# q and k of the last four attention tiles turned during the first batch, kept in device memory and loaded back

## What is computed

```python
for c in range(nc):                                   # attention, chunk = 32
    k_full = np.concatenate([mem_k, k_ctx], axis=2)   # 8 memory rows and the window
    v_full = np.concatenate([mem_v, v_ctx], axis=2)
    scores = scale * np.matmul(q_c, k_full.transpose(0, 1, 3, 2))
    a = softmax(scores)
    out[:, :, c_start:c_end] = np.matmul(a, v_full)
x = out as (3072, 512)
h = x @ w_in                                          # 512 -> 1024
solu = h * softmax(h)
ln = (solu - mean) / sqrt(var + 1e-6) * g_ln
x2 = ln @ w_out                                       # 1024 -> 512
h = x2 @ moe2_w_in                                    # 512 -> 2048
out = (h * clip(h + 3, 0, 6) / 6) @ moe2_w_out
```

## Time and profile before

| | us |
|---|---|
| median of 3 runs (908.24 to 909.01) | 908.4 |
| the profiled execution: its own time | 907.72 |
| the profiled execution: its span | 905.6 |
| first batch, to the first `project` | 0 to 73.7 |
| attention and first layer, with what overlaps them | 73.7 to about 410 |
| second layer | to the end |

### The profile page before, as it was taken

How to read it: one execution, slowest core, us unless ns; L and a number is a source line. 1 busy time by engine, 2 the same in 40 slices (tenths; PEclk the granted TensorE clock), 3 DMA queues, 4 the chain that set the end, 5 groups by cost and what they waited for, 6 DMA issues and landing times.

```text
span 905.6 us, 16510 instructions
## 1 busy us (share of the span) xinstructions
PE 887.2 (98%) x6144; PEld 794.8 (88%) x6144; DVE 676.9 (75%) x1100; ACT 470.7 (52%) x1092; POOL 265.9 (29%) x327
## 2 busy tenths in 40 slices
PE   7899999999999999999999999999999999999998
PEld 6778888888888888899888888888799999999998
DVE  5998878888777878757685555555898987979784
ACT  6666565656565565627574555455654333333321
POOL 4392554563431453450112233223510000000000
PEclk9999999999999999999999999999999999999999
DMA  9744266656554574558633323333997435354341
GB/s 206 167 96 107 57 187 177 187 155 184 148 153 119 149 214 123 190 205 314 253 126 140 128 104 139 134 142 117 337 351 268 145 95 162 95 162 140 117 140 47
DMA packets 147196, 146.70 MB, mean 162 GB/s; under 512 B 96952, under 2 KB 107704, under 8 KB 146104
## 3 DMA queue, kind: packets, MB, share of 16 engines
q1 hardware_dynamic: 133539, 100.29, 38.3%
q0 software_dynamic: 7920, 38.94, 11.9%
q10 hardware_dynamic: 5669, 6.56, 2.1%
HBM read 90.05 MB, written 55.71 MB: 161 GB/s over the span
## 4 chain that ended last, share of the span: by engine, by line
PE 85%; DVE 8%; DMA 3%; ACT 1%; issue 1%; SPq 0%; ACTq 0%; POOL 0%; DVEq 0%; POOLq 0%
PE banks L981 26%; PE banks L1270 23%; PE banks L1029 23%; PE banks L926 3%; PE banks L955 2%; PE banks L934 2%; PE banks L896 2%; PE banks L972 2%; PE banks L996 2%; DMA gs_raw<-g_scratch 2%; DVE prob L1640 1%; DVE gs L1601 1%; DVE small L1618 1%; DVE score L1610 1%; DVE gs_raw L1954 1%
## 5 line engine op out<-in xcount | busy, mean ns | idle before, releaser
L1270 PE MATMUL banks<-vs,gs 128*128 128x256 f32 x2016 | 242.9, 283 | 1.1 <-DVE o_stage L1998 0.7
L1270 PEld LDWEIGHTS banks<-vs,gs 128*128 128x128 f32 x2016 | 242.2, 192 | 1.8 <-DVE o_stage L1998 0.9
L1029 PE MATMUL banks<-xs,ws 128*128 128x512 f32 x1008 | 231.2, 390 | 0.6 <-DVE part L1729 0.3
L1029 PEld LDWEIGHTS banks<-xs,ws 128*128 128x128 f32 x1008 | 188.0, 188 | 42.5 <-issue 2.0
L1558 ACT CAST gs<-gs_raw 128x1792 fp32r<-128x1792 f32 x48 | 81.4, 1697 | 125.7 <-DVE gs_raw L1954 125.7
L981 PE MATMUL banks<-y_t,w_out 128*128 128x384 f32 x768 | 140.9, 338 | 0.0
L981 PEld LDWEIGHTS banks<-y_t,w_out 128*128 128x128 f32 x768 | 132.2, 188 | 0.7
L981 PE MATMUL banks<-w_in,x_t 128*128 128x512 f32 x480 | 114.5, 394 | 0.0
L1337 ACT ACTIVATE prob<-score,small 96x128 f32<-96x128 f32 x256 | 99.3, 392 | 16.6 <-DVE small L1618 16.1
L1954 DVE TENSOR_TENSOR gs_raw<-gs_raw 128x256 f32<-128x256 f32 x192 | 82.2, 429 | 31.6 <-DMA gs_raw<-g_scratch 26.8
L981 PEld LDWEIGHTS banks<-w_in,x_t 128*128 128x128 f32 x480 | 88.6, 188 | 18.7
(11 more groups left out here) (94 smaller groups left out, 1071.1 us busy)
## 6 DMA issues: line engine op xcount, KB each, us to landing
g_scratch<-part SPq DMA_DIRECT2D x96, 256.0 KB, 2.0
gs_raw<-g_scratch SPq DMA_DIRECT2D x45, 512.0 KB, 3.8
q_in<-in_q_dram SPq DMA_DIRECT2D x32, 192.0 KB, 4.4
x_scratch<-x_out ACTq DMA_DIRECT2D x32, 192.0 KB, 2.7
k_in<-in_k_dram SPq DMA_DIRECT2D x24, 240.0 KB
v_in<-in_v_dram SPq DMA_DIRECT2D x24, 240.0 KB
out_dram<-o_stage SPq DMA_DIRECT2D x11, 512.0 KB, 5.4
v_split_scratch<-v_split POOLq DMA_DIRECT2D x3, 1792.0 KB, 8.0
```

The lines of the kernel that those rows point to most:

```text
L1029: mm = pe.matmul(ps, ws[:, W_OF[i], a, kc, :], xs[g][X_OF[i]][:, m, kc, :], start=(fresh and x == 0), stop=(x == len(passes) - 1), skip_gr ...
L1270: mm = pe.matmul(m_ps[i][:, s, :], gs[x][:, a, G_OF[i], s * P:(s + 1) * P], vs[p][:, m, V_OF[i], :], start=(p == 0 and s == 0 and y == 0), ...
```

## The change

Tiles 28 to 31, the last four of the last batch, are called ahead (`is_ahead`, AHEAD = 4, e = 0 to 3). During the first batch SP loads their q and k into two slots of new buffers `q_raw` and `k_raw`, PE transposes them into bank 7 (`turn_ahead_q`, `turn_ahead_k`), ACT copies them out (`copy_ahead_q`, `copy_ahead_k`), and SP stores the turned tiles in device memory (`keep_ahead`). In the last batch SP loads the turned tiles into `q_back` and `k_back`, which lie where `q_in` and `k_in` lie, `scores` reads them from there, and `turn_qk` and `copy_qk` of these four tiles are gone. The first batch's orders are written anew on all five engines, and `keep_busy` has 23 matmuls there where it had 24. Five semaphores of fixed values become one (`fixed_ready`).

```diff
             def load_q(b, t):
                 n = TILES * b + t
-                if type(n) is not int or n >= 2:
+                if n >= 2 and is_ahead(n - 2):
+                    sp.wait_ge(scores_done, 2 * n - 2)
+                elif n >= 2:
                     sp.wait_ge(qk_turned, 2 * n - 3)
+                if is_ahead(n):
+                    sp.dma_start(q_back[t % 2][:, :, :], q_dram[n - NA + AHEAD]).then_inc(q_in_here[t % 2], 16)
+                    return
...
+            def load_ahead_q(e):
+                t = ahead_tile(e)
+                if e >= 2:
+                    sp.wait_ge(ahead_turned, 2 * e - 3)
+                sp.dma_start(q_raw[:, e % 2], q[B - 1, :, TQ * t:TQ * (t + 1), :].rearrange("h s d -> s h d")
+                             ).then_inc(raw_here[e % 2], 16)
+
+            def load_ahead_k(e):
+                if e >= 2:
+                    sp.wait_ge(ahead_turned, 2 * e - 2)
+                load_window(sp, k_raw, k, mem_k, raw_here, B - 1, ahead_tile(e))
+
+            def keep_ahead(e):
+                sp.wait_ge(ahead_copied, 2 * e + 2)
+                sp.dma_start(q_dram[e], q_ahead[:, e % 2]).then_inc(ahead_kept[e % 2], 16)
+                sp.dma_start(k_dram[e], k_ahead[e % 2][:, :, :]).then_inc(ahead_kept[e % 2], 16)
...
+                load_ahead_q(3)
+                keep_ahead(1)
+                keep_ahead(2)
+                load_ahead_k(3)
+                keep_ahead(3)
...
+            def turn_ahead_q(e):
+                pe.wait_ge(raw_here[e % 2], raw_count(e))
+                turn(ahead_ps, q_raw[:, e % 2], TQ, ahead_turned)
+
+            def turn_ahead_k(e):
+                turn(ahead_ps, k_raw[:, e % 2], NK, ahead_turned)
...
                 pe.wait_ge(y_lo_done, 2 * (turned_tile(i, 0) + [0, 1, 1, 2][u]))
+                if is_ahead(n):
+                    return
...
                 attend(0, 6, False)
+                pe.wait_ge(ahead_copied, 7)
+                turn_ahead_k(3)
                 pe.wait_ge(y_lo_done, 5)
                 pe.wait_ge(y_lo_done, 6)
+                pe.wait_ge(ahead_copied, 8)
...
-                    if not last:
+                    if not last and not is_ahead(n + 1):
                         copy_qk(n + 1)
```

More of the change, by code:

```diff
@@ L344, in work, with is_ahead, ahead_tile, raw_count @@
             }
+        IDENT_READY, THREE_READY, MASK_READY = 2, 3, 5
+        def is_ahead(n):
+            return n >= NA - AHEAD
+        def ahead_tile(e):
+            return TILES - AHEAD + e
+        def raw_count(e):
+            return 16 * sum(1 + LOADS[ahead_tile(x)] for x in range(e % 2, e + 1, 2))
+        def k_in_count(n):
+            b, t = n // TILES, n % TILES
+            return kv_here(b, t) - (16 * sum(LOADS[x] - 1 for x in range(TILES - AHEAD, t + 1) if x % 2 == t % 2) if is_ahead(n) else 0)
         def first_cols(m):
@@ L455, in _ @@
             for b in range(1, B):
+                if b == B - 1:
+                    for s in range(2):
+                        sp.wait_ge(ahead_kept[s], 16 * AHEAD)
                 batch(b)
@@ L835, in _ @@
             first_batch()
+            for s in range(2):
+                pool.wait_ge(ahead_kept[s], 16 * AHEAD)
             batch(1, steps=0, start=1)
@@ L892, in _, with turn @@
         def _(pe):
-            def turn(ps, src, width):
+            def turn(ps, src, width, turned=qk_turned):
                 for c in range(KD):
@@ L898, in turn @@
                                         ident[0:width, 0:width])
-                last.then_inc(qk_turned, 1)
+                last.then_inc(turned, 1)
             def turn_q(t, ps):
@@ L939, in turn_probs @@
                 for half in range(2):
-                    if behind_qk:
+                    if behind_qk and not is_ahead(n + 1):
                         pe.wait_ge(qk_copied, 2 * n + 3 + half)
-                    elif half == 0:
+                    elif not behind_qk and half == 0:
                         pe.wait_ge(y_lo_done, 2 * MPG * (NG - 1))
@@ L1113, in first_batch @@
                 turn_q(5, turn_ps[0])
+                turn_ahead_q(0)
                 hidden_part(1, 0)
                 hidden_part(1, 1)
-                hidden_part(1, 2)
                 pe.wait_ge(prob_copied, 8)
                 turn_k(5, turn_ps[1])
+                hidden_part(1, 2)
                 hidden_part(1, 3)
                 attend(0, 3, False)
-                scores(5, False)
                 pe.wait_ge(qk_copied, 11)
                 turn_half(4, 0)
+                scores(5, False)
+                pe.wait_ge(ahead_copied, 1)
+                turn_ahead_k(0)
                 pe.wait_ge(qk_copied, 12)
@@ L1133, in first_batch @@
                 hidden_part(2, 2)
-                hidden_part(2, 3)
                 pe.wait_ge(y_lo_done, 1)
                 turn_q(6, turn_ps[0])
+                hidden_part(2, 3)
                 pe.wait_ge(y_lo_done, 2)
                 turn_k(6, turn_ps[1])
+                pe.wait_ge(ahead_copied, 2)
+                turn_ahead_q(1)
+                attend(0, 4, False)
                 pe.wait_ge(qk_copied, 13)
@@ L1156, in first_batch @@
                 hidden_part(3, 3)
-                scores(7, False)
                 pe.wait_ge(qk_copied, 15)
@@ L1161, in first_batch @@
                 turn_half(6, 1)
+                scores(7, False)
                 pe.wait_ge(prob_copied, 13)
```

301 lines of the change are left out of this document (178 added, 123 removed).

## The result

| kernel | median | lowest to highest | runs |
|---|---|---|---|
| before | 908.7 us | 907.27 to 912.25 | 6 |
| changed | 916.61 us | 915.73 to 919.59 | 6 |

The ratio is 1.009, with a 95% interval of 1.0074 to 1.0105. The change makes the kernel 7.9 us slower; 5.0 were forecast. Direction and range held, and the size was 3 us low.

The account below looks back on a forecast made before the run. PE was taken as the bound, busy 98% of the span, with the first batch more DVE's. -3.1 + 1.0 + 0.4 + 1.6 + 5.1 = +5.0 us on 907.7 gave 912.7, as median 913.4 us; range 909 to 918.

Parts of the forecast that it names:

- taken out: Last batch, tiles 28 to 31: PE time without the q and k transposes falls by 3.1 us, bounds 2.2 to 3.3.
- ahead transposes, exposed: First batch: 1.0 us of six transpose groups exposed on PE, plus 0.4 for q of ahead tile 3.
- first wait: Before q of ahead tile 3: PE waits 1.6 us for k of ahead tile 3 to land, between 0 and 3.
- second wait: First batch's end: tile 8's loads, issued behind the ahead stores, make PE's k 5.1 us late, between 4.5 and 7.
- new order: First batch: rewritten engine orders and four more loads in full DMA queues, costed at 0, between -2 and +2 us.
- clock: Behind the second wait: PE's granted clock stays as it is, costing 0; this forecast got chance 0.52.
- rival 1: PE's clock falls behind the second wait, slowing `project`: +2.2 us, 915.6 us, up to 918; chance 0.22.
- Rival 2: First batch: the new order takes out 4 us of DVE's waiting, giving 906.8 us; chance 0.14.
- Rival 3: Last batch: the gain is lost, for example to late loads or DVE, giving 916.5 us; chance 0.06.
- Near 80: Sign at the first batch's end: the first `project` begins near 80 us instead of 73.7.

Follow-up runs that it names:

- f3: Kernel before, no ahead work put in, last batch as in the changed kernel but loading back stored zeros: 906.43 us, ratio 0.9974.
- e2: Changed kernel, loads of tile 8's q and k ahead of ahead tiles 2 and 3's stores, ahead tile 3's k ahead of all stores: 907.57 us, ratio 0.9992.
- e4: Changed kernel's new order on all engines, with all ahead work taken out and the last batch as before: 910.83 us, ratio 1.0024.
- e5: Changed kernel with the load of k of ahead tile 3 issued ahead of the stores of ahead tiles 1 and 2: 915.20 us, ratio 1.0071.
- e3_fill_wait: Changed kernel with 16 idle matmuls on PE behind the last ahead copy, before q of tile 8: 917.17 us, ratio 1.0091.
- e1_tile8_first: Changed kernel with loads of q and k of tile 8 issued ahead of the stores of ahead tiles 2 and 3: 911.69 us, ratio 1.0039.
- f4_wait_moved: f1_old_order_ahead with PE's wait for the last ahead copy moved from before q of tile 8 to before `project`: 907.92 us, ratio 0.9991.
- f1_old_order_ahead: Kernel before, its old order kept, with the ahead work put in and the last batch as changed: 907.79 us, ratio 0.9984.

## Why the prediction was right, and 3 us low

Term by term, each measured in single profiles, as a difference of two kernels that differ in little but that term:

| term | forecast | measured | from |
|---|---|---|---|
| taken out | -3.1 | -3.2 | attention stretch, f3 and e2 against before |
| ahead transposes, exposed | 1.0 + 0.4 | 1.7 | stretch, e2 - e4 |
| first wait | 1.6 | 1.6 | stretch, changed - e5 |
| second wait | 5.1 | 5.5 (0.4 of it the clock's) | stretch, e5 - e2 |
| new order | 0 | 1.6 | stretch, e4 - before |
| clock | 0 (rival 1: 2.2) | 1.0, and the 0.4 above | `project`, 5.43 - 4.43 |
| sum | 5.0 | 8.2 | 7.9 in whole runs |

The whole runs by themselves give: order 2.2, the work put in and taken out -2.9 (e2 against e4; the terms give 1.7 - 3.2 = -1.5), first wait 1.7, second wait with clock 7.2, together 8.2 us. Either sum closes by construction, since each kernel is subtracted from the next on the way from before to changed; only the single terms can be compared, and in whole runs each is uncertain by about 1.5 us or more.

**Taken out: right.** The step of tile 31 is 1.02 us shorter; 0.92 were forecast. With the slow `project` taken off, the changed kernel's attention stretch is 294.9 us, as in f3 and e2. What came back later can't be seen: f3 is 2.4 us faster in whole runs, with 3.2 within its interval.

**The first wait: right in its mechanism, its size in part by luck.** The chain that the prediction laid from the end of `turn_ahead_k(2)` to the landing was 5.1 us. In the trace that transpose ends about 68.5 and q is turned at 73.66: 5.1 us. PE had 3.4 us to do in it and waited 1.76. But e3_fill_wait, with the same list, took 5.9 us and waited 2.54, and in e1_tile8_first the wait is 3.19, each with the clock down behind it; taking the first wait away was worth 1.7 us of whole runs beside the second wait (changed against e5) and 4.1 without it (e1 against e2).

**The second wait: right in its mechanism and, in part by luck, in its size.** ACT and SP in the changed kernel, against the earlier trace rows:

```profile
79.75 1.07 ACT L1442 CAST y_t<-banks 128x512 fp32r<-128x512 f32 x2 [0.72 <-PE banks L1050]
80.71 1.13 ACT L1468 ACTIVATE h_exp<-banks,small 128x1024 f32<-128x1024 f32 x1
...
81.81 0.60 ACT L1424 COPY k_ahead<-banks 128x512 f32<-128x512 f32 x1
```

```profile
82.44 0.34 SPq L474 DMA_DIRECT2D q_ahead_scratch<-q_ahead  x1
82.82 0.43 SPq L475 DMA_DIRECT2D k_ahead_scratch<-k_ahead  x1
83.30 0.45 SPq L446 DMA_DIRECT2D q_in<-in_q_dram  x1
...
84.73 0.50 SPq L408 DMA_DIRECT2D k_in<-in_k_dram  x1
```

The chain from the casts is the one forecast: `exp_hidden(3)` 1.13 us, the copy 0.60, two stores 0.86, then the loads. The last piece of k went out 1.43 us behind q (1.18 forecast) and landed some 3.3 us later (2.8 forecast): 0.8 us more than the working had. As a difference of two kernels the wait comes to 5.5 us. It is not more, because e2_both_first, from which it is counted, turns k of tile 8 itself 0.7 us later behind ACT's casts than before did (2.15 us against 1.46), waiting for the last ahead copy. And 0.4 of the 5.5 are the clock's: from k of tile 8 to `project` are 0.77 us (88.09 to 88.86) where they are 0.36 in e2_both_first.

**The clock: the step that failed.** The forecast took the clock as it is at 0.52 and rival 1 at 0.22. Rival 1 holds: at 1.00 before the wait, 0.50 behind it, in the changed kernel and in e5_k3_first; with the wait filled, 1.00. The argument against it, that the trace of before shows no fall, was worth little, since PE is never idle there for more than 1.54 us behind its start, as the prediction itself says, and so it was no test of a wait of 5. With the 0.4 us on k of tile 8 the fall cost 1.4 us in the changed kernel's profile and 2.3 in e5_k3_first's (`project` 6.34 us), against the 2.2 of rival 1; in the changed kernel the clock comes back within `project`. No whole run shows this cost by itself, since e3_fill_wait came out no faster.

**The new order: the term that was mis-sized.** It was costed at 0, between -2 and +2, and it costs 1.6 us in the stretch and 2.2 in whole runs (0.7 to 3.7 by the interval). The 0 was the middle between two guesses, less waiting of DVE and later loads; what decides, where in its list PE meets DVE, was in neither. e4_order_only shows these meetings at 41.09, 50.35 and 64.18. Which engine's list makes them late is not shown: POOL's order and one transpose of PE were tried alone and changed nothing. Rival 2, that the new order pays, falls with it.

**The ahead transposes: nearly right.** 1.7 us for 1.4; in the old order 2.3, of which 0.5 is the wait for the last copy (f4_wait_moved against f1_old_order_ahead).

**The rest.** Rival 3 is refuted by the attention stretch; that its 916.5 us is nearly the measured time is luck, and so is rival 1's 915.6 in part, as it has no cost of the order. The first `project` begins at 88.86 us. "Near 80" was a slip of the prediction's: its own terms put 8.1 us ahead of it, which gives 81.8. Of the 7.0 us between, 2.3 are the terms that were too small and 4.8 the late start of this one profile, most of it the scaling of 3.83 us on DVE. No experiment ties it to the change, as the eight other profiles with the new order start at 36.34 to 38.75. What part of the start is the change's own is not settled; profiles of one execution each can't tell it.

Put together: of 8 us lost, 6.5 are one line too late in SP's list, with what the clock adds to it, 1.6 are another line there, and the rest of the change is about level: the order and the work put in cost 3.2 us and the work taken out gives 3.2 back.

## What to carry to other kernels

A queue that issues DMAs in order makes every load behind a waiting store as late as the store; a load with a deadline belongs ahead of it, and for a step that is moved the whole list of the issuing engine has to be read, not only that of the engine that computes. Work that is moved out of a full stretch into a less busy one gains its length and costs what the holes there don't hold, here 3.2 us against 1.7 for the work and 1.6 for the order written to make room for it. An idle time longer than any in the profile at hand should be priced with a fall of the clock behind it; here that was 1.4 and 2.3 us in two profiles.

## What the runs showed of the hardware that I had not expected

The clock also falls behind shorter idle times, in the first 38 us, where the DMA queues are full. In the changed kernel PE is idle for 2.56 us before 22.50 and for 3.34 us before 31.58:

```profile
22.50 0.87 PE L969 MATMUL banks<-ident,k_in 128*128 128x128 f32 x4 [2.56 <-DMA k_in<-in_k_dram]
...
31.58 0.52 PE L1022 MATMUL banks<-ident,prob 96*128 96x96 f32 x4 [3.34 <-DVE prob L1765]
```

```profile
8.00:38.00 30.00, 21.76 (x188) 18.78 (x189) 26.34 (x43) 17.55 (x71) 14.32 (x18) 0.89 1.11 236
20.00:24.00 4.00, 1.50 (x9) 1.53 (x10) 3.93 (x8) 1.84 (x9) 1.56 (x2) 0.84 1.13 270
```

Here no single idle time has to be that long. In f3_take_out_only, which has the old order, PE is idle for 1.42 us before 22.11 and for 1.49 before 26.12, the longest between 8 and 38 us, and no longer than the 1.54 us of before, behind which the clock stayed at 1.00. Yet it falls (time line of PE, then a window):

```profile
26.12 0.52 PE L1025 MATMUL banks<-ident,prob 96*128 96x96 f32 x4 [1.49 <-DVE prob L1743]
...
28.34 2.02 PE L1017 MATMUL banks<-k_t,q_t 64*96 64x128 f32 x16
```

```profile
28.00:32.00 4.00, 4.00 (x28) 3.22 (x25) 3.28 (x7) 2.13 (x9) 3.08 (x3) 0.61 0.96 161
```

The sixteen matmuls of the scores take 2.02 us here and 1.12 elsewhere. So a flat clock row in one profile doesn't say that the kernel is safe from a fall: the next execution can have it.

The mean granted clock from 8 to 38 us is 0.89 in the changed kernel and 1.00 in before, but also 0.89 in f1_old_order_ahead and 0.94 in f3_take_out_only, which have the old order. It does not set the start by itself: e1_tile8_first has 0.89 too and the earliest start, 36.34 us. The start, with DMA shares from 0.89 to 1.12, differs by up to 5.3 us between the 14 profiles (36.34 to 41.61 us for the scores of tile 4), which are of different kernels, and by 3.4 us between the changed kernel and e3_fill_wait, which are the same up to there. A single profile says nothing on a change of 2 us there.
